# Seven block products in place of eight for the second matrix of a two-layer MLP, in a fused attention, mixture and MLP kernel

## The chip, the cores and the metric

One core of a Trainium2 chip (trn2). The metric is the time of one execution on the device in microseconds (us), the median of three runs. The engines are PE (TensorE, matrix products into PSUM), DVE (VectorE), ACT (ScalarE), POOL (GpSimd, which reads and writes SBUF alone) and SP (SyncE, which here issues DMAs).

## What is computed

Three layers in a row, all in float32, for 2 sequences of 768 tokens: attention with a band of keys and a few global ones, an attention mixture of 4 experts of which each token takes 2, and a layer that mixes tokens at rank 32 and then runs an MLP with a residual.

```python
attn_out = _attn_ref(q, k, v, n_global, n_local)          # (2, 8, 768, 64)
x = attn_out.transpose(0, 2, 1, 3).reshape(B, S, 512)
x = _moe_ref(x, w_gate, wq, wk, wv, wo)                   # out = sum of gates * (a @ v @ wo[e])
# _moe2_ref
h = x.transpose(0, 2, 1) @ U @ V                          # rank 32 over the tokens
u = x + h.transpose(0, 2, 1)
ch = np.maximum(u @ w_ch1, 0.0) @ w_ch2                   # 512 -> 2048 -> 512
return u + ch
```

## The kernel before

Every large product of float32 values is made from halves: a value is split into a high part (a float32r copy) and a low part (value minus high part), and three products are added in PSUM: high by high, high by low, low by high. `split_product` (L1217) issues these three for each group; line L1220 is the matmul of all of them.

The program has three stretches. **Attention** (to some 94 us) works in 24 steps of two units ("duos"). In step d PE makes the scores of duo d (`scores`, L1239), the value products of duo d-3 (`values`, L1272) and the transposes of duo d-2 (`transposes`, L1252). DVE subtracts the bias (`attend`, L847), takes sums and inverses (L872, L878), evacuates three of four transposes (L865) and makes the low part of x (L885); ACT takes exponentials (L604), the fourth evacuation (L613) and the high part (L625); POOL divides (L541). The high and low parts of the first key weights are made by POOL before the steps, those of the first query weights by ACT (L638) and DVE (L908) in the steps' tail. **The mixture** (to some 221 us) goes through 24 units; POOL divides there too (L567) and, behind some units, splits blocks of wo and of w1 (`split_weight`, `split_w1`, both through `lo_of`, L492). In it and in the passage behind it (221 to 239 us) PE also makes wo times w1, in eight blocks `w01h`/`w01l`, so that the hidden layer can be made from the mixture's output directly.

**The MLP** (from 239 us to the end) is what the change rewrites. The hidden layer has 16 tiles of 128 rows for each of the 2 sequences, so f runs from 0 to 31. `hidden(f)` makes one tile for 768 tokens: 12 matmuls into ps_o, six of 128x512 and six of 128x256. ACT makes its high part with the rectifier (`hidh`, L796), DVE its low part from PSUM and `hidh` (`hidl`, L1203). The weights w2 come by DMA a tile at a time into `fraw` (L481); DVE casts them to `fh` (L1162, `f_hi`), and POOL makes `fl` (L492). `second(f)` adds the tile into the whole output of a sequence, which stays in six PSUM banks: 4 blocks of 128 rows by 512 and by 256 tokens, 24 matmuls. `whole(b)` adds wo times the mixture's output in the same way, worth two more such tiles for each sequence. PE's order is hidden(f+1), second(f), so ACT and DVE have the time of second(f) to make the next operand. At a sequence's end the banks are copied by DVE (L1198) and ACT (L790) and stored.

```python
            for f in range(B * FT):
                if f + 1 < B * FT:
                    hidden(f + 1)
                second(f)
                if f == FT - 1:
                    whole(1)
```

Of the kernel before, what the change touches and what calls it, by code (L numbers as in the profile page):

```python
# [21 lines left out]
P = 128  # L22
B, H, S, D = 2, 8, 768, 64
DM = H * D
# [12 lines left out]
FR = 3  # L37
# [10 lines left out]
LAST_PIECES = [(0, 0), (0, 1), (1, 1), (1, 0), (2, 0), (3, 0), (2, 1), (3, 1)]  # L48

DRAINS = [(0, 1, LO, 1), (0, 2, HI, 3), (1, 1, LO, 4), (2, 1, LO, 5), (3, 1, LO, 6), (2, 2, HI, None)]  # L50
DVE_DRAINS, ACT_DRAINS = (0, 2, 4), (1, 3, 5)
# [24 lines left out]
WO_BEHIND = {0: (10, 11), 1: (12, 13), VMIX_BEHIND: (14,)}  # L76

WK_0, WV, WQK_1, WO, VMIX = 2, 6, 10, 14, 15
# [52 lines left out]
def build(nc, t, out):  # L131
    ctx = ExitStack()
    with ctx:
# [17 lines left out]
        xh = sb("xh", [P, B, KT, S], F32R)  # L151
        xl = sb("xl", [P, B, KT, S], F32R)
        prob = sb("prob", [P, 4, S])
        soft = ExitStack()
        probT = sb("probT", [P, 2, 2, S], where=soft)
        soft.close()
        hidh = sb("hidh", [P, 2, S], F32R)
        hidl = sb("hidl", [P, 2, S], F32R)
# [11 lines left out]
        wv_h = sb("wv_h", [P, KT, 260], F32R)  # L170
        wv_l = sb("wv_l", [P, KT, 260], F32R)
        woT_h = sb("woT_h", [P, KT, 2 * P], F32R)
        woT_l = sb("woT_l", [P, KT, 2 * P], F32R)
        wo_h = sb("wo_h", [P, EP, DM], F32R)
        wo_l = sb("wo_l", [P, EP, DM], F32R)
        wraw = sb("wraw", [P, 2, 1040])
# [49 lines left out]
        w01_soon = sb("w01_soon", [P, 2, W1_IN_FILL, EP, W1N], F32R, where=exp_)  # L226
        exp_.close()
        mlp = ExitStack()
        fraw = sb("fraw", [P, 2, DM], where=mlp)
        fh = sb("fh", [P, FR, DM], F32R, where=mlp)  # L230
        fl = sb("fl", [P, FR, DM], F32R, where=mlp)
        w01_late = sb("w01_late", [P, 2, W1P - W1_IN_FILL, EP, W1N], F32R, where=mlp)
        y = prob
# [46 lines left out]
        wq_raw = wraw[:, 0, 0:KT * 256].rearrange("p (k n) -> p k n", k=KT)[:, :, P:2 * P]  # L280
# [4 lines left out]

        def two_hi(m):

            return ps_t[:, m // 2, :].rearrange("p (a n) -> p a n", a=2)

# [21 lines left out]
        wq_hi, wq_lo = sem("wq_hi"), sem("wq_lo")  # L311
# [7 lines left out]
        fh_done, fl_done, hid_done, hidh_done, hidl_done, fo_done = (  # L319
            sem(n) for n in ("fh_done", "fl_done", "hid_done", "hidh_done", "hidl_done", "fo_done"))  # L320
        acc_done, y_dve, y_act, y_out = sem("acc_done"), sem("y_dve"), sem("y_act"), sem("y_out")
# [21 lines left out]
        def _(sp):  # L343
# [42 lines left out]

            def load_late_weights():

                load_qk("wq", qk_first, P, 0, wq_in)
                load_wv()  # L390
                load_qk("wk", qk_raw, 0, 1, wqk_in)
                load_qk("wq", qk_raw, P, 1, wqk_in)
                sp.dma_start(wo_raw, t["wo"]).then_inc(wo_in, 16)
# [11 lines left out]
            load_qk("wk", qk_first, 0, 0, wk_in)  # L405
# [3 lines left out]
            with sp.If(is_narrow(sp)):  # L409
                for p in range(2, B * HP):  # L410
                    load_keys(p)
                    load_values(p)
                    if p == 3:
                        load_constants()
                    elif p == 4:
                        load_late_weights()
            with sp.Else():
                load_constants()
# [32 lines left out]
            def load_w1(j):  # L451

                if j == 0:
                    sp.wait_ge(wl_done, WK_0)
                    sp.wait_ge(wq_lo, 1)
# [1220 lines left out]
```

## Time and profile before

| | |
|---|---|
| runs, us | 458.44, 459.03, 459.30; median 459.03 |
| the profiled execution's own time, us | 458.41 |
| its span on the core, us | 456.6 |
| PE busy | 442.3 us, 97% of the span |
| DVE, ACT, POOL busy | 190.8, 167.1, 173.1 us |
| TensorE clock granted | full speed in all slices |
| DMA | 33.47 MB, 73 GB/s over the span |

The span is what the trace shows, from the core's first to its last instruction; the execution's own time has 1.8 us more around it. Matmuls overlap, so a matmul's own duration says little of its cost: what counts is the distance from one start to the next. The same holds, less strongly, for two instructions of DVE or ACT with no wait between them.

### The profile page before, as it was taken

What the parts mean: (1) busy time and instruction counts of PE and PEld (TensorE: products, weight loads), DVE (VectorE), ACT (ScalarE), POOL (GpSimd) and SP (SyncE); (2) the same over time, 40 slices, a digit from 0 to 9 for tenths busy, and PEclk for the clock granted to TensorE, in tenths of its full rate; (3) what the DMA queues carried; (4) which work ended last, traced back from release to release, by engine and by line L of the source; (5) the groups of instructions that cost most, each with busy time, mean ns of one, the idle gap of its engine ahead of it and who ended that gap; (6) DMA issues with size and microseconds to landing.
All of it is one profiled execution on the core that took longest, in us unless ns stands there. A gap on an engine that the chain in (4) does not pass through costs nothing.

```text
span 456.6 us, 8488 instructions
## 1 busy us (share of the span) xinstructions
PE 442.3 (97%) x3194; PEld 368.0 (81%) x3194; DVE 190.8 (42%) x616; ACT 167.1 (37%) x452; POOL 173.1 (38%) x243
## 2 busy tenths in 40 slices
PE   4999999999999999998999999999999999999996
PEld 3677777887787887767998888888888888888885
DVE  5799989455632733544352222212223122222112
ACT  4888788232553654656430111110112111111102
POOL 2667766924961365775212122222112111222210
PEclk9999999999999999999999999999999999999999
DMA  8899950110020011110102011111111032311003
GB/s 257 257 244 298 299 161 1 51 45 2 1 94 0 2 47 47 47 48 1 47 10 61 24 46 46 41 31 46 47 46 47 0 93 92 93 46 47 25 1 138
DMA packets 29949, 33.47 MB, mean 73 GB/s; under 512 B 9204, under 2 KB 19444, under 8 KB 29908
## 3 DMA queue, kind: packets, MB, share of 16 engines
q1 hardware_dynamic: 29474, 32.40, 24.0%
q8 instruction: 26, 0.43, 0.4%
q10 hardware_dynamic: 434, 0.52, 0.3%
q14 instruction: 15, 0.12, 0.1%
HBM read 29.77 MB, written 3.15 MB: 72 GB/s over the span
## 4 chain that ended last, share of the span: by engine, by line
PE 89%; DVE 4%; issue 3%; ACT 2%; DMA 1%; SPq 0%; POOL 0%; DVEq 0%; ACTq 0%
PE ps_s L1220 27%; PE ps_o L1220 25%; PE ps_t L1220 12%; PE ps_s L1451 5%; PE ps_o L1484 4%; PE ps_t L1467 4%; PE ps_o L1272 3%; PE ps_s L1239 3%; PE ps_t L1252 3%; DVE probT L865 1%; PE ps_o L1396 1%; ACT prob L604 1%; DMA kT<-in_k 1%; DVE prob L847 1%; DVE smin L847 0%
## 5 line engine op out<-in xcount | busy, mean ns | idle before, releaser
L492 POOL TENSOR_TENSOR fl<-fraw,fh 128x512 fp32r<-128x512 f32 x32 | 41.4, 1292 | 177.9 <-DVE fh L1162 177.9
L604 ACT ACTIVATE prob<-prob,smin 128x256 f32<-128x256 f32 (+3 forms) x144 | 77.7, 540 | 36.4 <-DVE smin L847 36.0
L796 ACT ACTIVATE hidh<-ps_o 128x768 fp32r<-128x768 f32 x32 | 26.0, 813 | 175.9 <-PE ps_o L1220 175.9
L1203 DVE SCALAR_TENSOR_TENSOR hidl<-ps_o,hidh 128x768 fp32r<-128x768 f32 x32 | 30.7, 958 | 92.6 <-ACT hidh L796 92.6
L541 POOL TENSOR_SCALAR prob<-prob,sinv,one 128x256 f32<-128x256 f32 (+1 forms) x96 | 50.6, 542 | 22.4 <-DVE sinv L878 22.4
L567 POOL TENSOR_SCALAR prob<-prob,sinv,gate 128x128 f32<-128x128 f32 (+5 forms) x48 | 34.0, 717 | 51.6 <-DVE sinv L898 51.5
L1220 PE MATMUL ps_s<-hidh,fl 128*128 128x512 f32 x128 | 50.4, 394 | 0.0
L1220 PE MATMUL ps_s<-hidl,fh 128*128 128x512 f32 x128 | 50.2, 392 | 0.0
L1220 PE MATMUL ps_s<-hidh,fh 128*128 128x512 f32 x128 | 49.7, 388 | 0.0
L1162 DVE CAST fh<-fraw 128x512 fp32r<-128x512 f32 x32 | 14.4, 450 | 66.8 <-PE ps_t L1220 66.8
L1220 PE MATMUL ps_o<-xh,w_late 128*128 128x512 f32 (+1 forms) x160 | 41.6, 334 | 0.0
L847 DVE CUSTOM_DVE_ANT_0 prob<-ps_s,bias 128x256 f32<-128x256 f32 (+1 forms) x96 | 34.5, 398 | 6.2 <-PE ps_s L1239 5.7
L847 DVE CUSTOM_DVE_ANT_0 prob<-ps_s,causal 128x128 f32<-128x128 f32 (+5 forms) x48 | 29.2, 615 | 18.7 <-PE ps_s L1451 11.8
L1220 PE MATMUL ps_t<-hidh,fh 128*128 128x256 f32 x128 | 35.3, 276 | 0.0
L1220 PE MATMUL ps_t<-hidl,fh 128*128 128x256 f32 x128 | 35.3, 276 | 0.0
L1220 PE MATMUL ps_t<-hidh,fl 128*128 128x256 f32 x128 | 35.3, 276 | 0.0
L684 ACT ACTIVATE probT<-ps_t 128x512 f32<-128x512 f32 (+1 forms) x48 | 24.2, 538 | 21.1 <-PE ps_t L1467 21.0
L1239 PE MATMUL ps_s<-kT,qT 64*128 64x256 f32 (+1 forms) x192 | 28.5, 423 | 3.0 <-DMA kT<-in_k 3.0
L1220 PEld LDWEIGHTS ps_o<-xh,w_late 128*128 128x128 f32 x160 | 28.5, 188 | 3.2
L1220 PEld LDWEIGHTS ps_t<-hidl,fh 128*128 128x128 f32 x128 | 24.0, 188 | 5.5
L1220 PEld LDWEIGHTS ps_t<-hidh,fh 128*128 128x128 f32 x128 | 24.0, 188 | 5.2
L1220 PEld LDWEIGHTS ps_s<-hidh,fl 128*128 128x128 f32 x128 | 24.1, 188 | 4.8
(182 smaller groups left out, 978.3 us busy)
## 6 DMA issues: line engine op xcount, KB each, us to landing
fraw<-in_w SPq DMA_DIRECT2D x32, 256.0 KB, 2.7
wraw<-in_w SPq DMA_DIRECT2D x8, 512.0 KB, 3.4
kT<-in_k SPq DMA_DIRECT2D x16, 224.0 KB, 4.1
vN<-in_v SPq DMA_DIRECT2D x8, 384.0 KB, 4.9
out<-prob SPq DMA_DIRECT2D x12, 256.0 KB, 2.8
qT<-in_q SPq DMA_DIRECT2D x7, 384.0 KB, 3.8
vB<-in_v SPq DMA_DIRECT2D x8, 192.0 KB, 4.8
kT<-in_k SPq DMA_DIRECT2D x7, 128.0 KB, 3.9
```

The source lines that it names most:

```text
L492: return pool.tensor_tensor(lo, raw, hi.bitcast(F32), ALU.subtract)
L541: pool.tensor_scalar(x, x, sinv[:, s:s + 1], one[:, 0:1], ALU.mult, ALU.mult).then_inc(norm_done, 1)
L567: pool.tensor_scalar(x, x, sinv[:, col + par:col + par + 1], gate[:, NT * b + i, e:e + 1], ALU.mult, ALU.mult).then_inc(mnorm_done, 1)
L604: act.activation(prob_s, prob_s, ACT.Exp, bias=smin[:, col:col + 1], scale=-1.0, accum_out=ssum[:, col:col + 1]).then_inc(done, 1)
L684: act.activation(flat[:, n0 * P:n1 * P], ps_t[:, g % 2, 0:(n1 - n0) * P], ACT.Copy).then_inc(mevac_done, 1)
L796: act.activation(hidh[:, f % 2, :], ps_o[:, 0:S], ACT.Relu).then_inc(hidh_done, 1)
L847: dve.tensor_tensor_reduce(out=dst, in0=src, in1=mask, scale=-SCALE, scalar=3e38, op0=ALU.add, op1=ALU.min, accum_out=smin[:, col:col + 1] ...
L1203: dve.scalar_tensor_tensor(hidl[:, f % 2, :], ps_o[:, 0:S], 0.0, hidh[:, f % 2, :].bitcast(F32), ALU.max, ALU.subtract).then_inc(hidl_done, 1)
L1220: last = pe.matmul(dst, a, m, start=start and k == 0, stop=stop and k == n - 1, **kw)
L1239: pe.matmul(a_score[s % 8][:, 0:keys.stop - keys.start], qT[half, p % 2, i * P:(i + 1) * P], kT[half, p % 2, keys], start=True, stop=True, ...
L1451: last = pe.matmul(ps_s[:, score_banks(2 * v + par)[0] + k, 0:z - a], mq[half, pp, i * P:(i + 1) * P], mk[half, pp, a:z], start=True, stop ...
L1467: last = pe.transpose(ps_t[:, g % 2, (n - n0) * P:(n - n0 + 1) * P], m_prob[(2 * v + par) % 6][:, j * P:(j + 1) * P], ident[:, :])
```

## The change

**The MLP's second matrix.** w2 (2048 rows) and wo (256 rows) are taken as one matrix of 2304 rows by 512 columns, its rows in 9 pairs of 256. The 1536 tokens of the two sequences are taken as 3 parts of 512. A pair's product for a part is then a product of a 2x2 matrix of 256x256 blocks (a11, a12, a21, a22) with another (b11, b12, b21, b22), and is made from seven block products instead of eight. For that, four sums of weight blocks (s1 to s4) and four sums of unit blocks (t1 to t4) are made first, and each of the seven products has a PSUM bank of its own, which gathers over the nine pairs of a part. At a part's end the seven banks are combined into the four output blocks (`sum_11`, `other_sums` on DVE, `sum_22` on POOL, two copies on ACT).

**Who makes what for a pair g.** DVE: s1 to s4 of pair g+2 (`weights_combined`), t1 to t4 of pair g+1 (`hidden_combined`), the low part of the three plain unit blocks (`hidden_lo`), the low part of the seven weight blocks (`weights_lo`). ACT: the rectifier of both hidden tiles into `hraw`, the high parts of the plain unit blocks, of the weight blocks and of the combined unit blocks. POOL: the low part of the combined unit blocks t1 to t4. All of DVE's and POOL's operands here are in SBUF. In front of the eight pairs of w2, the pair of wo takes its unit blocks from the mixture's output, so it has no hidden tiles.

**PE.** For a pair: the first hidden tile of the next pair, two products, the second hidden tile, five products. A part's last pair has no hidden tiles ahead of it. The products with t1 to t4 come behind the third place in the plain order and from the third place on in the first and last pair of a part.

**In front of the MLP.** The high and low parts of both first weights are now POOL's, between the divides of steps 13, 16, 19 and 22; their loads and those of the constants stand later in SP's queue; wo is no longer split on POOL behind the mixture's first units; in the attention, the value products come one step later (duo d-4), and so do `x_hi` and `x_lo`. In the passage before the MLP, DVE and ACT also make the blocks of pairs 0 and 1. The buffers are laid out anew.

```diff
+PRODUCTS = {1: ("a11", "b11"), 2: ("a12", "b21"), 3: ("s4", "b22"), 4: ("a22", "t4"), 5: ("s1", "t1"), 6: ("s2", "t2"),
+            7: ("s3", "t3")}
+ORDER, END_ORDER = (1, 2, 3, 5, 7, 6, 4), (1, 2, 6, 7, 5, 3, 4)
...
-WO_BEHIND = {0: (10, 11), 1: (12, 13), VMIX_BEHIND: (14,)}
-WK_0, WV, WQK_1, WO, VMIX = 2, 6, 10, 14, 15
+WK_0, WQ_0, WV, WQK_1, VMIX = 2, 4, 8, 12, 13
+SPLIT_AT = {13: 0, 16: 1, 19: 2, 22: 3}
...
 # SP
-                sp.dma_start(fraw[:, f % 2, :], t["w2"][f % FT]).then_inc(f_in[f % 2], 16)
+                if g >= 2:
+                    sp.wait_ge(al_done, g - 1)
+                if c and j == 4:
+                    store(c - 1)
+                src = t["w2"][2 * j - 2:2 * j].rearrange("f p n -> p f n") if j else t["wo"]
...
 # POOL, attention
                 for d in range(N_DUO + 1):
                     if 1 <= d <= N_DUO:
                         divide(d - 1)
+                    if d in SPLIT_AT:
+                        split_weight(SPLIT_AT[d])
...
 # POOL, MLP
-            for f in range(B * FT):
-                pool.wait_ge(fh_done, f + 1)
-                lo_of(fraw[:, f % 2, :], fh[:, f % FR, :], fl[:, f % FR, :]).then_inc(fl_done, 1)
+                pool.tensor_tensor(y22, u3, c5, ALU.add).then_inc(y22_done, 1)
+            for g in range(N_PAIR):
+                pool.wait_ge(bth_done, g + 1)
+                lo_of(t_raw, bt_hi[g % 2], bt_lo[g % 2]).then_inc(btl_done, 1)
+                if g and g % PAIRS == 0:
+                    sum_22(g // PAIRS - 1)
...
 # ACT, MLP
-            for f in range(B * FT):
-                act.activation(hidh[:, f % 2, :], ps_o[:, 0:S], ACT.Relu).then_inc(hidh_done, 1)
+            for g in range(N_PAIR):
+                if last_of_part(g):
+                    copy_of(g // PAIRS, 1, c1)
+                    if g + 1 < N_PAIR:
+                        combined_hi(g + 1)
+                    copy_of(g // PAIRS, 5, c5)
+                    if g + 2 < N_PAIR:
+                        weights_hi(g + 2)
+                else:
+                    hidden_out(g + 1, 0)
+                    hidden_out(g + 1, 1)
+                    hidden_hi(g + 1)
+                    if g + 2 < N_PAIR:
+                        weights_hi(g + 2)
+                    combined_hi(g + 1)
...
 # DVE, MLP
+            def weights_combined(g):
+                dve.tensor_tensor(s1, a21, a22, ALU.add).then_inc(s_step, 1)
+                dve.tensor_tensor(s3, a11, a21, ALU.subtract).then_inc(s_step, 1)
+                dve.wait_ge(s_step, 4 * g + 1)
+                dve.tensor_tensor(s2, s1, a11, ALU.subtract).then_inc(s_step, 1)
+                dve.wait_ge(s_step, 4 * g + 3)
+                dve.tensor_tensor(s4, a12, s2, ALU.subtract).then_inc(s_step, 1)
+            def hidden_combined(g):
+                if g:
+                    dve.wait_ge(btl_done, g)
+                dve.tensor_tensor(t1, b12, b11, ALU.subtract).then_inc(t_step, 1)
+                if is_hidden(g):
+                    dve.wait_ge(relu_done, 2 * hidden_before(g) + 2)
+                dve.tensor_tensor(t3_, b22, b12, ALU.subtract).then_inc(t_step, 1)
+                dve.tensor_tensor(t2, b22, t1, ALU.subtract).then_inc(t_step, 1)
+                dve.wait_ge(t_step, 4 * g + 3)
+                dve.tensor_tensor(t4, t2, b21, ALU.subtract).then_inc(t_step, 1)
+            def hidden_lo(g):
+                dve.wait_ge(b1h_done, hidden_before(g) + 1)
+                dve.tensor_tensor(b1_lo[g % 2], hraw[:, 1:4, :], b1_hi[g % 2].bitcast(F32),
+                                  ALU.subtract).then_inc(b1l_done, 1)
+            def weights_lo(g):
+                dve.wait_ge(ah_done, g + 1)
+                dve.tensor_tensor(a_lo[g % 3], fraw[:, g % 2, 1:8, :], a_hi[g % 3].bitcast(F32),
+                                  ALU.subtract).then_inc(al_done, 1)
...
+            for g in range(N_PAIR):
+                if g + 2 < N_PAIR:
+                    weights_combined(g + 2)
+                if g + 1 < N_PAIR:
+                    hidden_combined(g + 1)
+                if not last_of_part(g):
+                    hidden_lo(g + 1)
+                    if g + 2 < N_PAIR:
+                        weights_lo(g + 2)
+                else:
+                    sum_11(g // PAIRS)
+                    other_sums(g // PAIRS)
+                    if g + 2 < N_PAIR:
+                        weights_lo(g + 2)
...
 # PE
-                    if d >= 3:
-                        values(d - 3)
+                    if d >= 4:
+                        values(d - 4)
...
+            for g in range(N_PAIR):
+                order = END_ORDER if g % PAIRS in (0, PAIRS - 1) else ORDER
+                ahead = not last_of_part(g)
+                if ahead:
+                    hidden(g + 1, 0)
+                pe.wait_ge(al_done, g + 1)
+                for k, n in enumerate(order):
+                    if k == 2 and ahead:
+                        hidden(g + 1, 1)
+                    last = product(g, n)
```

On DVE, the MLP's steady order before was two instructions for a tile of 128 hidden rows. `fraw` is raw w2, `fh` its high part; `hidl` is the low part of a hidden tile.

```order
L1162 CAST fh<-fraw 128x512
L1203 SCALAR_TENSOR_TENSOR hidl<-ps_o,hidh 128x768
L1162 CAST fh<-fraw 128x512
L1203 SCALAR_TENSOR_TENSOR hidl<-ps_o,hidh 128x768
L1162 CAST fh<-fraw 128x512
```

Now, for a pair of tiles, it is ten. `t_mem` holds t1 to t4, `hraw` the rectified blocks, `b_parts` and `b_last` the parts of unit blocks, `a_third` and `a_third_low` one of the three places of the weight blocks.

```order
L1266 TENSOR_TENSOR fraw<-fraw 128x256
L1267 TENSOR_TENSOR fraw<-fraw 128x256
L1269 TENSOR_TENSOR fraw<-fraw 128x256
L1271 TENSOR_TENSOR fraw<-fraw 128x256
L1286 TENSOR_TENSOR t_mem<-hraw 128x256
L1289 TENSOR_TENSOR t_mem<-hraw 128x256
L1291 TENSOR_TENSOR t_mem<-hraw,t_mem 128x256
L1293 TENSOR_TENSOR t_mem<-t_mem,hraw 128x256
L1298 TENSOR_TENSOR b_parts<-hraw,b_parts 128x768
L1304 TENSOR_TENSOR a_third_low<-fraw,a_third 128x1792
```

The cast of the weights has gone to ACT; eight sums of blocks and the low part of the weights have come, and no operand of DVE's is in PSUM any more.

On POOL, at the passage from the mixture to the MLP, the order before was this:

```order
L581 CAST xh<-wraw 128x2x256
L492 TENSOR_TENSOR xl<-wraw,xh 128x2x256
L581 CAST xh<-wraw 128x2x256
L492 TENSOR_TENSOR xl<-wraw,xh 128x2x256
L492 TENSOR_TENSOR fl<-fraw,fh 128x512 x32
```

Now it is this:

```order
L652 CAST xh<-wraw 128x2x256
L566 TENSOR_TENSOR xl<-wraw,xh 128x2x256
L652 CAST xh<-wraw 128x2x256
L566 TENSOR_TENSOR xl<-wraw,xh 128x2x256
L566 TENSOR_TENSOR b_parts<-t_mem,b_parts 128x1024
L566 TENSOR_TENSOR b_last<-t_mem,b_parts 128x1024
```

32 subtractions of 512 columns on the weights have become 27 of 1024 columns on the combined unit blocks, the last two rows in turn.

## Rows read from the trace of the kernel before

**Rows 1.** The page, part 1: busy us, share of the span and instructions by engine.

```profile
PE 442.3 (97%) x3194; PEld 368.0 (81%) x3194; DVE 190.8 (42%) x616; ACT 167.1 (37%) x452; POOL 173.1 (38%) x243
```

**Rows 2.** Chain that ended last, in the MLP: start us, us, what.

```profile
239.38 2.05 PE ps_o L1220 x12
...
399.75 2.05 PE ps_o L1220 x12
...
405.91 2.05 PE ps_o L1220 x12
```

**Rows 3.** PE's timeline in the MLP and before it: start us, us, instruction.

```profile
236.47 0.28 PE L1220 MATMUL ps_s<-xh,woT_h 128*128 128x256 f32 x1
...
239.22 0.39 PE L1220 MATMUL ps_o<-xh,w_soon 128*128 128x512 f32 x1
...
401.64 0.39 PE L1220 MATMUL ps_s<-hidh,fh 128*128 128x512 f32 x1
...
402.33 0.28 PE L1220 MATMUL ps_t<-hidh,fh 128*128 128x256 f32 x1
...
405.75 0.39 PE L1220 MATMUL ps_o<-xh,w_late 128*128 128x512 f32 x1
...
452.86 0.28 PE L1220 MATMUL ps_t<-hidh,fl 128*128 128x256 f32 x1
```

**Rows 4.** DVE's timeline: subtractions with both operands in SBUF, and a chain of waits.

```profile
226.07 1.90 DVE L1091 TENSOR_TENSOR xl<-o,xh 128x512 fp32r<-128x512 f32 x3
...
238.16 1.82 DVE L1091 TENSOR_TENSOR xl<-o,xh 128x768 fp32r<-128x768 f32 x2
...
L1091 DVE TENSOR_TENSOR xl<-o,xh x5: 684/693/951, 226.1 to 239.0; 128x512 fp32r<-128x512 f32 x3, 128x768 fp32r<-128x768 f32 x2
...
106.01 0.26 DVE L1033 TENSOR_TENSOR geq<-geq,tie 128x96 f32<-128x96 f32 x1
106.31 0.26 DVE L1034 TENSOR_TENSOR ggt<-ggt,geq 128x96 f32<-128x96 f32 x1
```

**Rows 5.** POOL's line L492 by form: duration ns min/median/max.

```profile
L492 POOL TENSOR_TENSOR fl<-fraw,fh x32: 1287/1292/1304, 236.6 to 437.3; 128x512 fp32r<-128x512 f32 x32
...
L492 POOL TENSOR_TENSOR wqk_l<-nat,wqk_h x4: 727/736/740, 90.1 to 93.6; 128x256 fp32r<-128x256 f32 x4
```

**Rows 6.** Timelines where DVE and POOL overlap: a cast, and what POOL did.

```profile
240.40 1.30 POOL L492 TENSOR_TENSOR fl<-fraw,fh 128x512 fp32r<-128x512 f32 x1 [2.47 <-DVE fh L1162]
...
239.90 0.42 DVE L1162 CAST fh<-fraw 128x512 fp32r<-128x512 f32 x1
...
240.83 1.15 DVE L1162 CAST fh<-fraw 128x512 fp32r<-128x512 f32 x1
```

**Rows 7.** The same for DVE's TENSOR_TENSOR with two operands in SBUF.

```profile
150.87 0.85 POOL L567 TENSOR_SCALAR prob<-prob,sinv,gate 128x512 f32<-128x512 f32 x1
...
151.28 0.55 DVE L1033 TENSOR_TENSOR geq<-geq,tie 128x96 f32<-128x96 f32 x1
...
81.19 0.68 DVE L908 TENSOR_TENSOR wqk_l<-wraw,wqk_h 128x512 fp32r<-128x512 f32 x1
...
81.17 1.06 POOL L541 TENSOR_SCALAR prob<-prob,sinv,one 128x256 f32<-128x256 f32 x1
...
L541 POOL TENSOR_SCALAR prob<-prob,sinv,one x8: 551/553/1057, 79.5 to 83.8; 128x256 f32<-128x256 f32 x8
```

**Rows 8.** ACT's timeline at the start of the MLP.

```profile
239.42 0.60 ACT L705 ACTIVATE w_late<-ps_s 128x512 fp32r<-128x512 f32 x1 [1.89 <-PE ps_s L1220]
241.47 0.81 ACT L796 ACTIVATE hidh<-ps_o 128x768 fp32r<-128x768 f32 x1 [1.46 <-PE ps_o L1220]
```

**Rows 9.** DVE's timeline in the passage: its last piece of w01 there.

```profile
240.23 0.69 DVE L1073 TENSOR_TENSOR w_late<-ps_s,w_late 128x512 fp32r<-128x512 f32 x1
```

**Rows 10.** Windows of the attention: us, busy us of PE, PEld, DVE, ACT, POOL, clock, DMA.

```profile
20.00:40.00 20.00, 18.98 (x198) 14.35 (x194) 18.18 (x84) 17.38 (x66) 12.86 (x26) 1.00 0.92 236
40.00:60.00 20.00, 19.43 (x201) 14.51 (x201) 17.74 (x80) 16.23 (x63) 14.28 (x28) 1.00 0.87 256
```

More of the change, by code:

```diff
@@ L932, in _ @@
                 head_bias(0)
-                for d in range(N_DUO + 4):
+                for d in range(N_DUO + 5):
                     if 3 <= d < N_DUO + 3:
@@ L1606, in _ @@
-            hidden(0)
-            whole(0)
-            for f in range(B * FT):
-                if f + 1 < B * FT:
-                    hidden(f + 1)
-                second(f)
-                if f == FT - 1:
-                    whole(1)
+                w = slice(f * P, (f + 1) * P)
+                (b0, first), (b1, last) = tokens(c, 0), tokens(c, 1)
+                pieces = ([(b0, slice(first.start, last.stop), ps_o[:, 0:TOKENS])] if b0 == b1 else
+                          [(b0, first, ps_o[:, 0:BLOCK]), (b1, last, ps_o[:, BLOCK:TOKENS])])
@@ new lines, in hidden, with empty @@
+                for b, cols, dst in pieces:
+                    done = split_product(dst, [(w01h[j - 1][:, k, w], w01l[j - 1][:, k, w], oph[b][:, k, cols],
+                                                opl[b][:, k, cols]) for k in range(EP)], skip_group_check=True)
+                done.then_inc(hid_done, 1)
+            def empty(c, n):
+                if c:
+                    if n in (1, 5):
+                        pe.wait_ge(copy_done, 2 * c - (n == 1))
+                    if n != 1:
+                        pe.wait_ge(sum_step, SUMS * (c - 1) + {2: 1, 6: 2, 7: 3, 5: 4, 3: 5, 4: 6}[n])
+                elif n <= 4:
+                    pe.wait_ge(w01l_done, W1P - 4 + n)
+                else:
+                    pe.wait_ge(sum_done, OP_PIECES[1])
@@ new lines, in product @@
+            def product(g, n):
+                c, j = divmod(g, PAIRS)
+                a, b = PRODUCTS[n]
+                if j == 0:
+                    empty(c, n)
+                if b[0] == "t":
+                    pe.wait_ge(btl_done, g + 1)
+                    x = B_SLOTS[b] - 3
+                    mh, ml = bt_hi[g % 2][:, x, :], bt_lo[g % 2][:, x, :]
+                elif j:
+                    pe.wait_ge(b1l_done, hidden_before(g) + 1)
+                    x = B_SLOTS[b]
+                    mh, ml = b1_hi[g % 2][:, x, :], b1_lo[g % 2][:, x, :]
+                else:
+                    mh, ml = (op_block(x, c, int(b[1]) - 1, 2 - int(b[2])) for x in (oph, opl))
+                for m in range(2):
+                    w = slice(m * P, (m + 1) * P)
+                    last = split_product(banks[n][:, m * BLOCK:(m + 1) * BLOCK],
+                                         [(a_hi[g % 3][:, A_SLOTS[a], w], a_lo[g % 3][:, A_SLOTS[a], w], mh, ml)],
+                                         start=j == 0 and m == 0, stop=last_of_part(g), skip_group_check=True)
+                return last
```

380 lines of the change are left out of this document (202 added, 178 removed).

## The prediction

> **What bounds the kernel now.** Read the busy times first [rows 1]: PE is busy for 97% of the span, the others for 37 to 42%. Busy time of matmuls overlaps, so the chain that ended last comes next [rows 2]: from 239.4 us on it never leaves PE, and the same 12 matmuls into ps_o come back 6.16 us apart (399.75, 405.91), one tile's time, with nothing of another engine between them. The timeline gives prices [rows 3]. One second(f) runs from 401.64 to 405.75, 4.11 us for 12 matmuls of 512 and 12 of 256 columns. Its first three, of 512, take 0.69 us, so 0.229 each; three of 256 take a third of (4.11/4 - 0.69), 0.114 each. A 256 costs half a 512: there is no fixed price per matmul. Even 24 of 256 in a row (236.47 to 239.22) take 0.115 each. The MLP is thus bound by columns on PE, from 239.2 to 453.1, 213.9 us, and what lies behind its last matmul is 3.5 us.
>
> **PE's work, new.** A pair's seven products are 7 x 2 x 3 = 42 matmuls of 256, 42 x 0.114 = 4.78 us; 27 pairs are 129.1. Before, 32 tiles and the four tiles' worth of wo were 36 x 4.11 = 148.0. The hidden layer keeps its columns: 32 x 2.05 = 65.7 before, 48 tiles x 6 x 0.229 = 65.9 now, counted as equal. PE saves 18.9 us of the MLP, if it never waits. With its two hidden tiles (1.37 each) a pair has 7.52 us; a part's last pair has 4.78.
>
> **DVE's work, new.** All its subtractions now have both operands in SBUF. Three such of 512 take 1.90 us with the last at 0.69, so they start 0.605 apart; two of 768 take 1.82 with the last at 0.95, so 0.87 apart [rows 4]. That is 0.265 per 256 columns: 0.34 for one of 256, 1.93 for 1792. Where one waits for the result just before it, the next starts 0.04 behind the reported end [rows 4], so 0.34 + 0.08 + 0.04 = 0.46. A pair has six at 0.34, two at 0.46, one of 768 and one of 1792: 2.96 + 0.87 + 1.93 = 5.76 us. Alone that fits into 7.52. **POOL's**: 0.74 us for 256, 1.29 for 512 [rows 5], so 2.40 for 1024. **ACT's**: 0.60 for 512, 0.81 for 768 [rows 8], so 1.02 for 1024 and 1.65 for 1792; a pair has 2 x 0.60 + 0.81 + 1.65 + 1.02 = 4.7. No engine is over the 7.52 by itself.
>
> **But DVE and POOL do not work side by side.** A cast of DVE's that takes 0.42 took 1.15 when POOL was inside an L492 subtraction: it began 0.42 before its end, at 241.56, when POOL (240.40 to 241.70) was just done [rows 6]. The new instructions are no casts, so two other places matter more [rows 7]. A TENSOR_TENSOR of 96 columns with both operands in SBUF took 0.55 for 0.26 while POOL was at work until 151.72. The other way round, a divide of POOL's took 1.06 for 0.55 when DVE's two-operand subtraction L908 started 0.02 us behind it. So either engine waits for the other's whole instruction. The handover comes 0.14 us before POOL's reported end (241.56 against 241.70), and POOL begins at 81.17 + 1.06 - 0.55 = 81.68, 0.10 before DVE's 81.19 + 0.605. The Trainium skill, page "SBUF — State Buffer", section "Who interferes with whom", says that a DVE instruction with two SBUF inputs contends with a GpSimd instruction that reads SBUF, while one with a single SBUF input does not. By that rule nothing contended in the old MLP but the cast, and all ten instructions of the new one do; [rows 7] agree in both directions.
>
> So DVE and POOL form one ring for each pair: 5.76 + 2.40 - 0.14 - 0.10 = **7.92 us**, against PE's 7.52. It is a true cycle: t1 of the next pair waits for POOL's low part of this one, since they share t_mem; the order within it does not change its length. Bounds for it: no exclusion at all leaves PE's 7.52; reported durations without any overlap give 8 x 0.42 + 0.95 + 2.01 + 2.40 = 8.72. I take 7.92, as each start distance is a measured one. ACT's work lies beside the ring.
>
> **PE's waits, piece by piece.**
> - Start. In the passage DVE gets 8 sums, two of 1792 columns and loses three casts: some 2.96 + 3.86 - 1.2 = 5.6 us, of which part falls into its idle stretches, and POOL's first 2.4 us hold it up once. Its last piece of w01 moves from 240.9 [rows 9] to about 244.4. PE needs it at 239.2 + 1.37 + 4.1 + 1.37 = 246.0: no wait. Behind it come sums and low parts (5.76) and POOL's 2.3, so t-blocks of pair 1 are there at 252.5. PE wants them at 239.2 + 4.78 + 4 x 1.37 + 3 x 0.68 = 251.5. **+1.0**.
> - Inside the parts, 20 distances of ring against PE: 20 x 0.40 = **+8.0**.
> - Part ends, twice. From POOL's start on the last pair to its start on the next part's second pair the ring has: POOL 2.3, sums of two pairs 2.96, ACT's high part 1.1 with its hops, POOL 2.4 and its y22 about 1.1 (DVE's six output sums from PSUM lie beside these), low part of weights 1.9, eight sums 2.96, low parts 0.9 and 1.9. That is 17.5. PE has 4.78 + 7.52 = 12.3. 2 x 5.2 = **+10.4**.
> - The last pair wants its t-blocks after two products: **+1.0**.
>
> Together 20.4 us of waits against 18.9 us saved: the MLP is 1.5 us longer. The end (one sum of 512, one store) is like the old one.
>
> **The rest.** In the attention, DVE is busy for 0.91 and 0.89 of two windows and PE for 0.95 and 0.97 [rows 10]; PE's 1.6 idle us there are for the most part waits for evacuations that a value product one step later takes away. Against this, POOL gets four splits (0.40 + 0.74 each) between divides; it is busy for 13 to 14 of 20 us, so a later divide may come 0.4 late once or twice. I take -1.5; bounds -3 and +1.5. In the mixture POOL loses the splits of wo, 4 x 1.15 us, under a busy PE: 0. Loads moved in SP's queue: the first keys keep their place, 0. The doubled w2 loads wait for the low part of two pairs before and have a ring's time, 7.9 us: 0.
>
> Sum: +1.5 - 1.5 = 0 on the span; own time 458.4, and as the median of the runs shown lies 0.6 above the profiled execution, **458.9 us**. A change under 0.2%, 0.9 us, can't be told from none.
>
> **Rivals.**
> - **The ring as worked out** (forecast, 0.62): 458.9. Each 0.1 us on the ring moves the time by 2.4 (20 pairs and two at either part end). With the ring between 7.6 and 8.15: 451 to 464.5.
> - **No exclusion** (0.12), only casts and single-operand forms block. Then only a part's last pair waits: 0.60 + 0.81 + 1.65 + 1.02 + 2.4 = 6.5 against 4.78 of cover, 1.7 twice, and the start's 1.0: 4.4 of waits for 18.9 saved, with the attention's -1.5: 459.0 - 16.0 = **443**. For it: two rows are thin evidence. Against it: they show both directions.
> - **The ring is looser** (0.26), the slower side: DVE and POOL swap once or twice more per pair, or the early handovers don't hold for long instructions. From 8.0 us on per pair it is slower than before. At 8.2 it costs 0.28 x 24 = 6.7: **465.6**. At the upper bound 8.72 it is 478. The Trainium skill, page "VectorE: DVE Perf Modes", section "The DRAIN you can't avoid", says that the next DVE instruction doesn't start until the pipe is empty; by it eight short ones would take their full durations and the ring would be near the upper bound. The start distance of 0.605 at a length of 0.69 speaks against that [rows 4], so I leave 0.04 of the 0.26 to it.
>
> **Numbers.** Forecast cases: 0.32 faster, 0.11 within 0.2%, 0.19 slower; no exclusion: 0.12 faster; looser ring: 0.02 faster, 0.02 same, 0.22 slower. Sum 0.46, 0.13, 0.41. The range 447 to 466 holds the forecast's own (451 to 464.5) and the looser ring up to 8.2; it leaves out no exclusion and the upper bound.
>
> **What would show it.** Right: in the new MLP POOL's subtraction of 1024 columns is reported at well over 2.4 us (it waits inside), DVE's short sums right behind it too, POOL's starts recur each 7.9 us, PE waits at products 5 to 4 for POOL, and longest at part ends; PE's matmul starts stay 0.114 apart. Wrong: PE without gaps inside parts and POOL at 2.4 (no exclusion); starts on POOL over 8.1 apart (looser); waits on ACT or DMA, which I cost at nothing; or attention that ends later than 94 us.

## The result and the profile after

The changed kernel takes 460.44 us (median of 17 runs, 458.66 to 461.31), the kernel before 458.44 in the same runs (17, 456.94 to 459.49): a ratio of 1.0042, with a 95% interval of 1.0029 to 1.0055. It is slower by 1.9 us, where no change was forecast. The span went from 456.6 to 458.9.

The page, part 1, of the changed kernel, to be read beside [rows 1]:

```profile
PE 434.0 (95%) x3464; PEld 372.4 (81%) x3464; DVE 353.9 (77%) x830; ACT 260.7 (57%) x545; POOL 230.5 (50%) x237
```

PE's 434.0 is 8.3 us less than before; the same matmuls come to 424.8 in the last experiment below, where they wait less, so some 9 us of its waits, and of a stretch at a lower clock (below), are counted as busy. DVE's share has gone from 42% to 77%, POOL's from 38% to 50%, and part of both is waiting, as the next views show.

POOL's timeline in the new MLP (start us, us, instruction, in brackets its idle time before and who ended it): the steady distance, and then the end of a part.

```profile
262.21 3.80 POOL L566 TENSOR_TENSOR b_last<-t_mem,b_parts 128x1024 fp32r<-128x1024 f32 x1 [4.17 <-ACT b_parts L871]
270.19 3.80 POOL L566 TENSOR_TENSOR b_parts<-t_mem,b_parts 128x1024 fp32r<-128x1024 f32 x1 [4.18 <-ACT b_parts L871]
...
302.09 3.73 POOL L566 TENSOR_TENSOR b_parts<-t_mem,b_parts 128x1024 fp32r<-128x1024 f32 x1 [4.17 <-ACT b_parts L871]
309.86 2.44 POOL L566 TENSOR_TENSOR b_last<-t_mem,b_parts 128x1024 fp32r<-128x1024 f32 x1 [4.04 <-ACT b_parts L871]
312.26 1.31 POOL L669 TENSOR_TENSOR y<-sums 128x512 f32<-128x512 f32 x1
319.69 3.79 POOL L566 TENSOR_TENSOR b_parts<-t_mem,b_parts 128x1024 fp32r<-128x1024 f32 x1 [6.11 <-ACT b_parts L871]
```

One and the same subtraction is reported at 3.80 us inside a part and at 2.44 at a part's end, where DVE makes its six sums from PSUM (308.61 to 312.90): inside, 1.4 us of it are waiting. Its starts recur 7.98 us apart, and 302.09 to 319.69 is 17.60.

DVE's timeline over the same round:

```profile
269.68 2.02 DVE L1304 TENSOR_TENSOR a_third_low<-fraw,a_third 128x1792 fp32r<-128x1792 f32 x1
271.61 2.66 DVE L1266 TENSOR_TENSOR fraw<-fraw 128x256 f32<-128x256 f32 x1
274.19 0.41 DVE L1267 TENSOR_TENSOR fraw<-fraw 128x256 f32<-128x256 f32 x1
274.53 0.41 DVE L1269 TENSOR_TENSOR fraw<-fraw 128x256 f32<-128x256 f32 x1
...
277.65 2.02 DVE L1304 TENSOR_TENSOR a_low<-fraw,a_mem 128x1792 fp32r<-128x1792 f32 x1
279.59 2.66 DVE L1266 TENSOR_TENSOR fraw<-fraw 128x256 f32<-128x256 f32 x1
```

POOL's instruction starts at 270.19, while DVE is inside the 1792-column one; it ends at 270.19 + 3.80 = 273.99 and takes 2.42 where nothing holds it up (at 233.32, before the MLP), so its work begins at 271.57. DVE's short sum, 0.42 alone, is issued at 271.61 and reported at 2.66: it ends at 274.27, so its work begins at 273.85. The two engines hand over to each other twice in a round, once in each direction, and nothing else stands in it: 271.61 to 279.59 is 7.98. The first of DVE's next sums, L1266, waits for nothing that POOL makes, so what holds it up is no signal. It is the ring of the forecast.

PE's timeline: the first matmul of the MLP and the last, to be read beside those of [rows 3].

```profile
236.70 0.39 PE L1389 MATMUL ps_o<-xh,w_soon 128*128 128x512 f32 x1
...
453.53 0.28 PE L1389 MATMUL ps_s<-b_parts,a_third_low 128*128 128x256 f32 x1
```

From start to start the MLP has 216.8 us, against 452.86 - 239.22 = 213.6 before: +3.2. It begins 2.5 us earlier. Behind the start of the last matmul come 5.4 us, against 3.7 before: +1.6. That is the whole difference of the spans, -2.5 + 3.2 + 1.6 = +2.3.

TensorE's granted clock was at its lower level, 0.50 of full speed, from 379.1 to 382.5, about where PE's wait of 2.39 us at the second part end is over (379.30), and at full speed over the first part end:

```profile
380.00:382.00 2.00, 2.00 (x11) 2.00 (x11) 1.93 (x6) 0.00 (x0) 0.00 (x0) 0.50 0.04 12
```

It costs the changed kernel nothing there, since the ring sets the pace: POOL's starts are 17.60 apart over the first part end and 17.58 over the second (375.54 to 393.12). Where PE sets the pace, as in some of the experiments, it does cost.

Windows of the end of both kernels (columns as in [rows 10]), first the changed one, then the one before:

```profile
455.00:457.00 2.00, 0.00 (x0) 0.00 (x0) 0.34 (x1) 0.00 (x0) 0.00 (x0) 1.00 0.68 223
457.00:458.90 1.90, 0.00 (x0) 0.00 (x0) 0.00 (x0) 0.00 (x0) 0.00 (x0) 0.66 0.53 179
```

```profile
451.00:453.00 2.00, 2.00 (x13) 1.69 (x11) 1.20 (x2) 0.69 (x2) 0.00 (x0) 1.00 0.82 287
453.00:455.00 2.00, 0.14 (x2) 0.00 (x0) 0.19 (x1) 0.60 (x1) 0.00 (x0) 1.00 1.02 374
```

Before, the stores flow from 451 on, while PE still works. Now three of the last part's four stores have to wait for the last sums, DVE's (until 455.34) and POOL's (until 454.60), and only then move. From the end of the last sum to the end of the span it is 3.56 us, where it was 2.82 behind ACT's last copy before (453.78 to 456.6).

The chain of waits of the changed kernel, its last pieces, shows why the sums themselves are late:

```profile
451.76 0.69 PE ps_o L1389 x6
...
452.56 0.61 ACT sums L880
...
453.25 0.70 DVE sums L1332
...
454.05 0.69 DVE y L1335
454.74 0.60 DVEq L172
```

Product 5 is whole at 452.5; a copy by ACT stands between it and DVE's sum, and DVE's last three sums follow in a row.

### The profile page after: what moved, and what is told of

It reads as the page before. It is cut to its first block and busy times, and to the rows that moved or that the text cites. A ratio compares the mean times of both kernels' runs of the same rounds, so it can differ in the third digit from the quotient of the medians.

```text
span 458.9 us, 9411 instructions
## 1 busy us (share of the span) xinstructions
PE 434.0 (95%) x3464; PEld 372.4 (81%) x3464; DVE 353.9 (77%) x830; ACT 260.7 (57%) x545; POOL 230.5 (50%) x237
## 5 line engine op out<-in xcount | busy, mean ns | idle before, releaser
L566 POOL TENSOR_TENSOR b_parts<-t_mem,b_parts 128x1024 fp32r<-128x1024 f32 x14 | 49.0, 3503 | 71.3 <-ACT b_parts L871 71.3
L566 POOL TENSOR_TENSOR b_last<-t_mem,b_parts 128x1024 fp32r<-128x1024 f32 x13 | 48.0, 3692 | 62.4 <-ACT b_parts L871 62.4
L856 ACT ACTIVATE hraw<-ps_o 128x512 f32<-128x512 f32 x48 | 28.7, 599 | 59.9 <-PE ps_o L1389 59.9
L1266 DVE TENSOR_TENSOR fraw<-fraw 128x256 f32<-128x256 f32 x27 | 61.3, 2271 | 0.2 <-DMA fraw<-in_w 0.2
L871 ACT ACTIVATE b_parts<-t_mem 128x1024 fp32r<-128x1024 f32 x27 | 28.2, 1044 | 12.4 <-DVE t_mem L1293 12.4
L684 ACT ACTIVATION_READ_ACCUMULATOR prob<-prob,smin 128x1 f32 x144 | 26.9, 187 | 0.0
L1421 PE MATMUL ps_t<-ident,prob 128*128 128x128 f32 x176 | 26.2, 290 | 0.7 <-POOL prob L611 0.7
L1389 PE MATMUL ps_o<-xh,w_soon 128*128 128x512 f32 (+1 forms) x96 | 26.3, 336 | 0.6 <-ACT hraw L856 0.6
L1389 PE MATMUL ps_s<-b_parts,a_third 128*128 128x256 f32 x136 | 25.4, 279 | 1.5 <-DVE b_parts L1298 1.5
L1389 PE MATMUL ps_o<-xl,w_late 128*128 128x512 f32 (+1 forms) x80 | 26.7, 334 | 0.0
L1636 PE MATMUL ps_t<-ident,prob 128*128 128x128 f32 x168 | 24.1, 276 | 1.1 <-ACT probT L756 1.1
```

The costliest lines, as they stand in the source:

```text
L566: return pool.tensor_tensor(lo, raw, hi.bitcast(F32), ALU.subtract)
L684: act.activation(prob_s, prob_s, ACT.Exp, bias=smin[:, col:col + 1], scale=-1.0, accum_out=ssum[:, col:col + 1]).then_inc(done, 1)
L856: act.activation(hraw[:, 2 * f:2 * f + 2, :], ps_o[:, 0:TOKENS].rearrange("p (s n) -> p s n", s=2), ACT.Relu).then_inc(relu_done, 1)
L871: act.activation(bt_hi[g % 2], t_raw, ACT.Copy).then_inc(bth_done, 1)
L1266: dve.tensor_tensor(s1, a21, a22, ALU.add).then_inc(s_step, 1)
L1389: last = pe.matmul(dst, a, m, start=start and k == 0, stop=stop and k == n - 1, **kw)
```

## Experiments

All ratios are to the kernel before, run beside each; 1.0042 is the changed kernel's own. Spans are of one profiled execution.

**1. Values a step later, alone, and undone.** In the kernel before, and reversed in the changed one:

```diff
-                    if d >= 3:
-                        values(d - 3)
+                    if d >= 4:
+                        values(d - 4)
```

(with `x_hi`, `x_lo` and the four first projections moved along by a step)

> The kernel before with one part of the change alone: the attention's value products (and with them x_hi, x_lo and the first projections) one step later. Nothing else is moved. Theory (the attention's gain is this part's): the mixture starts 2.6 us earlier than before, as it does in the changed kernel, and all of it reaches the end, 458.4 - 2.6 = 455.8 us. Rival (the gain is from POOL's splits or the loads that stand later in SP's queue): no change, 458.4.

> The changed kernel with the value products back at three steps behind (x_hi, x_lo four). Theory: +2.6 us, 463.0. Rival (the gain comes from elsewhere): 460.4. The MLP's length, 217 us from its first matmul, is as in the changed kernel by both.

Alone: 0.9957 (0.9929 to 0.9985), span 455.5. Undone: 1.0112 (1.0079 to 1.0144), span 460.9. The transposes of wo, behind the attention, begin at 92.80 before, 91.78 with the step alone, 92.12 with the step undone and 90.21 in the changed kernel. So the step is worth 1.0 us in the old surroundings and 1.9 in the new, and the other edits to the attention 0.7 to 1.6, each a difference of two profiled executions. PE's waits in the value products (from 20 to 92 us) say the same: 1.8 us before, none with the step, and 3.0 in the changed kernel without it. The view of PE's waits of that run:

```profile
PE ps_o L1441 <- DVE probT L978: 2.1, 6, 0.8
PE ps_o L1441 <- ACT probT L693: 0.9, 3, 0.4
```

The theory gave the step all 2.6; the runs give it 1.0 to 1.9 of them. Which of the other edits (POOL's splits between the divides, the order of the loads) has the rest was not tried. What the attention gains reaches the end undiminished: 1.0 earlier there, 1.1 on the span.

**2. More work for POOL that nobody waits for.** An extra subtraction of 256 columns on a dead buffer behind each of POOL's:

```diff
                 lo_of(t_raw, bt_hi[g % 2], bt_lo[g % 2]).then_inc(btl_done, 1)
+                if g:
+                    pool.wait_ge(extra, g)
+                pool.tensor_tensor(causal[:, 256:512], causal[:, 0:256], causal[:, 512:768],
+                                   ALU.subtract).then_inc(extra, 1)
```

> The changed kernel; POOL makes one more subtraction of 256 columns (0.74 us alone) for every pair, on a buffer that nobody uses any more, behind its signal, so that nobody waits for it. It computes nothing that is wanted. Theory (DVE and POOL exclude each other and form a ring of 7.98 us per pair): the ring grows by 0.74 - 0.24 = 0.50, times 20 pairs and two at each of two part ends, +12 us, 472.5; POOL's 1024-column subtractions recur 8.48 apart. Rival (POOL's reported 3.80 us is only its own slowness or a wait for data, and POOL has 2 to 4 us idle in each pair): no change, 460.4.

1.0347 (1.0304 to 1.0389), span 472.8: +13.9 us. POOL's timeline:

```profile
264.07 3.78 POOL L567 TENSOR_TENSOR b_last<-t_mem,b_parts 128x1024 fp32r<-128x1024 f32 x1 [3.84 <-ACT b_parts L876]
267.82 0.92 POOL L677 TENSOR_TENSOR causal<-causal 128x256 f32<-128x256 f32 x1
272.58 3.77 POOL L567 TENSOR_TENSOR b_parts<-t_mem,b_parts 128x1024 fp32r<-128x1024 f32 x1 [3.85 <-ACT b_parts L876]
```

Starts 8.51 apart, where 8.48 was expected. POOL still stands idle for 3.8 us in each round, and work that no instruction waits for costs 0.53 us of every round all the same (8.51 - 7.98). An idle engine whose work isn't free: this is shared access, not POOL's capacity.

**3. POOL out of the round.** DVE makes the low part of the combined blocks as well:

```diff
-            for g in range(N_PAIR):
-                pool.wait_ge(bth_done, g + 1)
-                lo_of(t_raw, bt_hi[g % 2], bt_lo[g % 2]).then_inc(btl_done, 1)
...
+            def combined_lo(g):
+                dve.wait_ge(bth_done, g + 1)
+                dve.tensor_tensor(bt_lo[g % 2], t_raw, bt_hi[g % 2].bitcast(F32), ALU.subtract).then_inc(btl_done, 1)
...
                     if g + 2 < N_PAIR:
                         weights_lo(g + 2)
+                    combined_lo(g + 1)
```

> The changed kernel with the low part of the four combined unit blocks made by DVE in place of POOL; POOL keeps only y22. Theory (ring by exclusion): DVE has 5.76 + 4 x 0.265 + 0.04 = 6.86 us for a pair and nothing to wait for, so inside the parts PE's 7.52 bounds: 20 x (7.98 - 7.52) = -9.2. At the two part ends DVE has 8 sums 2.96, low part 1.1, five output sums 3.2, low part of the weights 1.9, and then a pair of 6.86: 16.0 in place of 17.6, -1.6 each. -12.4 in all: 448. Rival (the bound is DVE's own work, because its short sums take their reported 0.42 us each): 8 x 0.42 + 0.95 + 1.23 + 2.01 = 7.55 with hops, about 8 per pair: 460. Rival (no exclusion, the loss is elsewhere): DVE only gets more work, 460 or above.

0.9845 (0.9799 to 0.9891), span 448.4; in a second series 0.9838 (0.9811 to 0.9865). More work on the busiest helper engine makes the kernel 2.0% faster than the changed one and 1.6% faster than the one before. DVE's timeline over one round:

```profile
268.68 1.22 DVE L1300 TENSOR_TENSOR b_parts<-t_mem,b_parts 128x1024 fp32r<-128x1024 f32 x1
269.81 0.42 DVE L1262 TENSOR_TENSOR fraw<-fraw 128x256 f32<-128x256 f32 x1
...
276.24 1.22 DVE L1300 TENSOR_TENSOR b_last<-t_mem,b_parts 128x1024 fp32r<-128x1024 f32 x1
```

The 1024 columns take DVE 1.13 us of its time (268.68 to 269.81), the sum behind them is back at 0.42, and the round is 7.56. DVE now has idle time in it, and PE has none: its waits in the whole MLP are

```profile
PE ps_s L1394 <- DVE b_parts L1294: 4.5, 2, 2.2
PE ps_t L1394 <- DVE b_parts L1300: 1.6, 1, 1.6
PE ps_t L1394 <- DVE b_last L1300: 1.6, 1, 1.6
```

all of them at part ends. The gain on the span, 10.5, is 1.9 short of the estimate. The trace shows two causes, which no run separates. DVE stood another 1.13 us at each part end, for ACT's high part. And the clock was at its lower level from 386.3 to 389.7, behind PE's wait of 2.23 us at 385.01; PE's matmuls of 512 columns started 0.43 apart, where 0.23 is usual. PE's timeline, and the window:

```profile
386.60 0.63 PE L1394 MATMUL ps_o<-xh,w_soon 128*128 128x512 f32 x1
387.03 0.63 PE L1394 MATMUL ps_o<-xl,w_soon 128*128 128x512 f32 x1
```

```profile
387.00:388.00 1.00, 1.00 (x4) 0.77 (x3) 1.00 (x2) 0.00 (x0) 0.00 (x0) 0.50 0.25 85
```

3.4 us at half the clock are 1.7 us of PE's work, an estimate from these starts. DVE's next three rounds there take 23.3 us, and 21.3 at the same place of the part before.

**4. The same extra work for POOL, where DVE has room.** In the kernel of experiment 3:

```diff
             for g in range(N_PAIR):
                 pool.wait_ge(bth_done, g + 1)
+                if g:
+                    pool.wait_ge(extra, g)
+                pool.tensor_tensor(causal[:, 256:512], causal[:, 0:256], causal[:, 512:768],
+                                   ALU.subtract).then_inc(extra, 1)
```

> The kernel in which DVE makes the low part of the combined unit blocks, and POOL makes for each pair one subtraction of 256 columns that nobody wants or waits for, at the same signal of ACT's as the extra one in the changed kernel, where it cost 14 us. Theory (POOL costs what it holds DVE up, and that only where DVE has nothing to spare): DVE's round of 6.9 grows to some 7.4 and stays under PE's 7.56; inside the parts nothing, +0.5 at either part end and at the start: +1.5 us, 0.987 of the kernel before. Rival (DVE is at its limit here as well, and 7.56 is its round and not PE's): +0.5 for every pair, +12, 1.010.

0.9872 (0.9842 to 0.9902), span 451.3: +2.4 to 2.9 us against the two runs of experiment 3, where the same 27 instructions had cost 13.9. DVE's and POOL's timelines:

```profile
254.73 1.76 DVE L1308 TENSOR_TENSOR b_parts<-t_mem,b_parts 128x1024 fp32r<-128x1024 f32 x1
256.42 0.41 DVE L1270 TENSOR_TENSOR fraw<-fraw 128x256 f32<-128x256 f32 x1
...
262.15 1.76 DVE L1308 TENSOR_TENSOR b_last<-t_mem,b_parts 128x1024 fp32r<-128x1024 f32 x1
```

```profile
260.72 2.10 POOL L676 TENSOR_TENSOR causal<-causal 128x256 f32<-128x256 f32 x1 [5.31 <-ACT b_parts L875]
```

POOL holds DVE up by 0.54 (1.76 for 1.22) in every round, and waits 1.36 itself; DVE's round is 7.42, and PE's 7.5 hides it. The cost shows at the part ends, where DVE is late, and part of it is the clock's: here it was at its lower level for 3.4 us behind both part ends (from 316 and from 388), in experiment 3 behind the second alone. By the estimate above that is 1.7 of the 2.4 to 2.9, so some 0.7 to 1.2 are left for the delay at the part ends, where 1.5 was expected. Whether the longer waits brought on the lower clock, no run shows. Experiments 2 and 4 together settle that what POOL costs is DVE's time, and that in the changed kernel DVE's round had none to give.

**5. The end.** The last part's y22 is made by DVE from the bank, first of the sums behind product 5, and stored second; ACT's copy and POOL's sum fall away there:

```diff
-                dve.wait_ge(copy_done, 2 * c + 2)
+                if c < PARTS - 1:
+                    dve.wait_ge(copy_done, 2 * c + 2)
                 dve.wait_ge(sum_step, SUMS * c + 3)
+                if c == PARTS - 1:
+                    dve.tensor_tensor(y22, banks[5], u3, ALU.add).then_inc(y22_done, 1)
```

> The changed kernel with another end of the last part alone: DVE makes y22 straight from the bank of product 5, as the first of the sums behind it, so ACT's copy of that bank and POOL's sum of 1.3 us fall away there, and y22 is stored ahead of y12. Theory (the end is 1.7 us longer than before because three of the four stores come within 0.7 us and stand in line for the DMA engines): y22's store starts some 1.5 us earlier, and the last result 0.3 us earlier; the stretch behind the last matmul falls from 5.2 to some 4.0 us, -1.2 us on the span. Rival (the stretch is the latency of the last result and its store, whatever the others do): -0.3.

> The changed kernel, unaltered, beside the runs of this series: 1.004 of the kernel before, as the first time.

1.0021 (1.0004 to 1.0038) beside 1.0041 (1.0019 to 1.0063) for the unaltered kernel of the same series. The intervals overlap; the traces are clearer. Behind the start of the last matmul come 458.6 - 453.92 = 4.7 us, in place of 5.4: -0.7, between the two expectations. From the end of the last sum to the end of the span it is 2.75 in place of 3.56, as only two stores are left in the line; the last sum itself came no earlier, since DVE has one more to make. In the kernel before, this stretch was 2.82. So about half of the 1.6 was the line of stores, 0.7. The other 0.9 stands ahead of the last result: 1.81 us from the start of the last matmul (453.53 to 455.34), 0.92 before (452.86 to 453.78), with DVE's sums in a row.

**6. Towards a better kernel.** Experiment 3 left PE's waits at the part ends. Three versions, each on top of the one before it.

> The kernel in which DVE makes the low part of the combined unit blocks, unaltered, beside the others of this series: 0.985 of the kernel before, as the first time.

> The kernel in which DVE makes the low part of the combined unit blocks, with three more edits. (1) That low part (and on ACT the high part) comes ahead of the weights' own: the wait of 1.6 us at the third product of the first and second part's last pair goes. (2) For the first pair of the second and third part it is POOL's, while DVE adds up the banks from PSUM: if operands in PSUM don't contend, POOL takes 2.4 us and DVE's sums stay 0.61 apart, and DVE comes 2.3 us earlier (1.23 and a wait of 1.13), so that PE's wait of 2.24 us behind each part end goes. (3) The end as in the run of the end alone, -1.2. Sum: 3.2 + 4.5 + 1.2 = 8.9 less than without them, some 0.966 of the kernel before. Rival: PSUM operands contend as well; then POOL's subtraction is held up over five sums (over 3.5 us) and DVE's first sum too, and half of the 4.5 stays: 0.971.

0.9874 (0.9846 to 0.9902), span 449.4: no better than experiment 3. Its first edit, on ACT in every pair, and likewise on DVE; and the second, on POOL:

```diff
+                    combined_hi(g + 1)
                     if g + 2 < N_PAIR:
                         weights_hi(g + 2)
-                    combined_hi(g + 1)
...
+            for c in range(PARTS - 1):
+                g = PAIRS * (c + 1)
+                pool.wait_ge(bth_done, g + 1)
+                lo_of(t_raw, bt_hi[g % 2], bt_lo[g % 2]).then_inc(btl_done, 1)
+                sum_22(c)
```

DVE's timeline:

```profile
290.68 1.23 DVE L1307 TENSOR_TENSOR b_last<-t_mem,b_parts 128x1024 fp32r<-128x1024 f32 x1 [0.27 <-ACT b_parts L873]
292.28 2.03 DVE L1312 TENSOR_TENSOR a_third_low<-fraw,a_third 128x1792 fp32r<-128x1792 f32 x1 [0.37 <-ACT a_third L849]
...
298.37 1.23 DVE L1307 TENSOR_TENSOR b_parts<-t_mem,b_parts 128x1024 fp32r<-128x1024 f32 x1 [0.26 <-ACT b_parts L873]
```

A wait of PE's of 1.6 us that came twice was traded for two short ones of DVE's, 0.27 and 0.37, in every pair: a round of 7.69, and DVE's again. Behind a part end PE's wait only changed its cause, 2.16 us for ACT's first hidden tile (at 308.71 and 379.88) in place of 2.24 for DVE. What did hold is the part on PSUM operands. POOL's 1024 columns lay beside DVE's sums from PSUM, and neither was held up, but the y22 that follows held up DVE's next subtraction of two SBUF operands by 0.64:

```profile
305.44 0.68 DVE L1332 TENSOR_TENSOR sums<-ps_t,sums 128x512 f32<-128x512 f32 x1
306.22 0.69 DVE L1335 TENSOR_TENSOR sums<-ps_t,sums 128x512 f32<-128x512 f32 x1
...
309.05 2.66 DVE L1312 TENSOR_TENSOR wqk_l<-fraw,wqk_h 128x1792 fp32r<-128x1792 f32 x1
```

```profile
306.16 2.41 POOL L569 TENSOR_TENSOR b_last<-t_mem,b_parts 128x1024 fp32r<-128x1024 f32 x1 [90.84 <-ACT b_parts L873]
308.50 1.33 POOL L672 TENSOR_TENSOR y<-sums 128x512 f32<-128x512 f32 x1
```

The next version keeps the new order to two pairs of a part:

```diff
+def soon(g):
+    return last_of_part(g + 1) or (g > 0 and g % PAIRS == 0)
...
+                    if soon(g):
+                        combined_hi(g + 1)
                     if g + 2 < N_PAIR:
                         weights_hi(g + 2)
-                    combined_hi(g + 1)
+                    if not soon(g):
+                        combined_hi(g + 1)
```

> The run of the low parts and the ends again, with what held it up taken out. There, ACT made the high part of the combined blocks ahead of the weights' in every pair, and DVE stood 0.27 and 0.37 us for ACT in each: a round of 7.68 against PE's 7.52. Now this order stands only in a part's last pair but one and in the first pair behind a part end; elsewhere it is the order of the changed kernel. Behind a part end ACT takes out the first hidden tile ahead of the weights' high part (PE waited 2.16 us for it), and DVE makes the unit blocks of the next pair ahead of the next weights' sums. Theory: rounds of 7.56, -0.12 x 18 = -2.2; -1.5 at either part end, -3.0: 449.4 - 5 = 444 on the span, 0.975 of the kernel before. Rival (DVE's work at a part end, 15 us for PE's 12.3, sets it in whatever order): -2.2 alone, 0.981.

0.9773 (0.9748 to 0.9797), between the two expectations; the MLP, from its first matmul to the start of its last, has 443.30 - 237.44 = 205.9 us. The last version gives ACT the hidden tile first there, too, and makes y22 from the bank at every part end:

```diff
                         combined_hi(g + 1)
+                    if g and g % PAIRS == 0:
+                        hidden_out(g + 2, 0)
                     if g + 2 < N_PAIR:
                         weights_hi(g + 2)
...
-                sum_22(c)
```

> The last kernel with what its trace still showed at the part ends taken out: behind the first pair of a part, too, ACT takes out the next hidden tile ahead of the weights' high part (PE waited 1.94 us), and DVE makes y22 from the bank of product 5 at all three part ends, so that POOL's sum of 1.3 us no longer holds up DVE's low part of the weights (2.69 us in place of 2.03) and ACT's copy goes. Theory: -1.9 at both, the 0.66 and DVE's own 0.6 cancel: -3.8, 0.969 of the kernel before. Rival (DVE is late there by its own work, so PE's wait only moves to DVE's result): 0.977 as the last one.

0.9698 (0.9667 to 0.973), span 443.8: 3.0% faster than the kernel before and 3.4% faster than the changed one. The MLP has 439.15 - 236.57 = 202.6 us, 14.2 less than in the changed kernel. Not all of the last step is the new order's: the version before it had the clock at its lower level from 388.1 to 391.5, where a round took 8.76 us, against 7.27 at the same place of the part before. This one has full clock in the whole MLP, so by the estimate of experiment 3 some 1.7 of the 3.3 us between 205.9 and 202.6 are the clock's. The page:

```profile
PE 424.8 (96%) x3464; PEld 366.7 (83%) x3464; DVE 335.7 (76%) x858; ACT 256.9 (58%) x542; POOL 134.5 (30%) x209
```

The same matmuls, and POOL at 30%. DVE is busy for less time than in the changed kernel (353.9) with more to do, since it no longer waits for POOL inside its instructions.

## Why the prediction was wrong, point by point

- **What bounds, and the saving on PE.** Right. In experiment 3, where PE shows no wait inside the parts, the steady rounds are about 7.56 us in the first and third part and 7.48 in the second, against 7.52. The forecast put nothing on the clock; that was right for the changed kernel, where the ring hides it; in experiment 3 it isn't hidden.
- **DVE and POOL exclude each other and form a ring.** Right, and the main point. The rival without exclusion falls by POOL's 3.80 and by experiments 2 and 4. So does the ring of 8.72 from full durations: DVE's short sums start 0.34 apart (274.19, 274.53) at a reported 0.41. The Trainium skill, page "SBUF — State Buffer", section "Who interferes with whom", says that two SBUF inputs on DVE contend with a GpSimd instruction that reads SBUF, and that an instruction with at most one doesn't, outside DVE's 2-port modes. The trace agrees in both directions, and POOL's 2.41 us beside DVE's sums from PSUM agree too.
- **Its size.** The first step that failed: "5.76 + 2.40 - 0.14 - 0.10 = 7.92". In the round shown above DVE works from 273.85 to 279.59, 5.74 as worked out, and POOL gives up 0.14 before its end, as worked out. But POOL begins 0.04 before DVE issues its next instruction (271.57 against 271.61), and not 0.10: 5.74 + 2.42 - 0.14 - 0.04 = 7.98. The 0.10 came from a divide of 256 columns [rows 7], the only pair of rows in that direction, and was rounded down besides: 81.795 - 81.68 is 0.115. Twenty distances inside parts (246.26 to 302.09, 319.69 to 375.54, 393.12 to 441.00) sum to 159.56 us, 1.2 more than at 7.92. The forecast said that each 0.1 on the ring moves the time by 2.4, and that from 8.0 on the kernel is slower: a result that turns with a few hundredths of a us in a round should have had less than its 0.13 for "no change" and more for either side.
- **Part ends.** Right: 17.60 and 17.58 for 17.5.
- **The start.** Right: POOL is done with pair 1 at 250.06, 13.4 us behind the MLP's first matmul, for 252.5 - 239.2 = 13.3.
- **The end.** The second step that failed, and the largest: "the end (one sum of 512, one store) is like the old one". It was 1.6 us longer. Only the last instruction was counted, and not what stands in line with it: three sums of DVE's behind product 5 and its copy, one more on POOL, and three stores of 256 KB that move only then. Before, the DMA engines had been at it since 451.
- **The attention.** The third, a size that was off: -1.5 forecast, -2.5 measured at the MLP's first matmul, within the bounds of -3 and +1.5. The waits of the value products were its source, as argued, but the row that was read for it gave them as "1.6 idle us", and the other edits of the attention brought 0.7 to 1.6 more (experiment 1).
- **Costs set at nothing** (loads, w01's last pieces, w2's transfers). Right: DVE waits 0.2 us for w2 in all, PE never for w01.

By the spans: MLP +3.2 for +1.5, end +1.6 for 0, attention -2.5 for -1.5; 2.3 in place of 0. Of the 1.7 that the MLP is over its forecast, 1.2 are the ring's inside the parts and 0.2 the part ends'; 0.3 stay unassigned. That the forecast came within 2 us is in part luck: the MLP and the end were put 3.3 too low, and the attention, 1.0 too high, took a third of it back. Had only the end been right, the forecast would have been slower by 1.6.

## What to carry to other kernels

Work on GpSimd is free only beside the right instructions of VectorE's. Here it was beside sums with one operand in PSUM (2.41 us on GpSimd, 0.68 and 0.69 for the sums, as alone), and wasn't beside instructions with two operands in SBUF, nor beside the cast of [rows 6]. Where both engines work on two SBUF operands, add their times as if they were one engine, less the short overlap of the handovers (5.74 + 2.42 - 0.18 = 7.98), and compare that sum with TensorE's. A subtraction that costs GpSimd 2.4 us costs VectorE 1.13, so the nominally idle engine was the wrong place for it. And price a program's end as a chain of its own: all the sums behind the last product and all the stores that then stand in line, not the last of each.

## What the runs showed of the hardware that was not expected

- An engine that waits for the other is reported as busy: 3.80 us for 2.42 on POOL, 2.66 for 0.42 on DVE. The waits view has nothing of it, DVE has next to no idle time in the ring, and the share of busy time overstates both.
- The handovers are not symmetric: DVE begins 0.14 us before POOL's reported end, while POOL begins 0.13 before DVE's reported end and only 0.04 before DVE could have issued its next instruction.
- In each of the rounds inside parts POOL is already waiting when DVE issues its next instruction behind the 1792 columns, and POOL goes first: DVE's one takes 2.66 us in place of 0.42. What decides it was not tested.
- Within the MLP the lower clock came in stretches of 3.4 us, each near the end of a wait of PE's of about 2 us, but not behind all such waits: in the changed kernel behind the second part end and not the first, with 2.39 and 2.40 us of waiting, and in experiment 3 likewise, with 2.23 and 2.24.
